# Two groups of a layer accumulated into one second product, GpSimd's work of a layer's first group in another order, a third softmax buffer, and copies of weights and values on ScalarE

## The chip, the cores and the metric

The kernel runs on one core of a Trainium2 chip. The time is device microseconds (us) of one execution, and the median of three runs is what is compared. TensorE (PE) multiplies matrices, VectorE (DVE), ScalarE (ACT) and GpSimd (POOL) work elementwise, SyncE (SP) issues all DMAs here. Each engine works through its own instructions in the written order and waits on semaphores for what others have to finish.

## What is computed

```python
def _attn_ref(q, k, v):                      # 4 x 8 heads, 576 positions, head size 64
    window = 128
    scores = 1.0 / np.sqrt(D) * np.matmul(q, k.transpose(0, 1, 3, 2))
    ...
    mask = (rel >= 0) & (rel < window)
    scores = np.where(mask, scores + bias[None], -1000000000.0)
    scores = scores - np.max(scores, axis=-1, keepdims=True)
    attn = np.exp(scores)
    attn = attn / (np.sum(attn, axis=-1, keepdims=True) + 1e-09)
    return np.matmul(attn, v)

def _moe_ref(x, w_gate, w_val, w_out):       # 2304 tokens, 512 -> 1536 -> 512
    gate = 1.0 / (1.0 + np.exp(-(x @ w_gate)))
    val = x @ w_val
    return gate * val @ w_out

def _moe2_ref(x, w1, w2, w3, w_out):         # 512 -> 1024 -> 1024 -> 512
    a = x @ w1
    b = x @ w2
    h = a * b @ w3
    return h @ w_out
```

The output is `_moe2_ref(_moe_ref(attention))`, in float32. Below, the two feed-forward parts are called layer 1 and layer 2.

## The kernel before

Every float32 operand is split into a high part (`..._hi`, the value cast to the type that PE multiplies quickly, made on ACT) and a low part (`..._lo`, value minus high part, made on DVE or POOL), and a product is three matmuls: high by high, low by high, high by low (`product`, L573).

**Head, 0 to about 134 us.** Attention for the first third of the tokens, 28 steps in `SLOTS` = 36 slots. A step n goes `scores` (PE), `score` (DVE: bias, mask and maximum, from PSUM into `soft[n % 2]`, `negmax`), `exponentials` (ACT), `reciprocals` (DVE), `normalise` (POOL, on `soft`), `turn` (PE: transposes), `turned_hi`/`turned_lo` (ACT, DVE), `pv` (PE: times the values), `out_copy` (ACT). The same slots multiply w3 by layer 2's w_out once (64 `fold`s of three matmuls, L634) so that layer 2 needs one product less; w3 comes in 16 halves, each cast to `w3_hi` on DVE (L1099), its low part from DVE (L1103) or POOL (L1325) in turn. `values_hi` (L981, L983) is on DVE too. The last eight folds follow the slots.

**Body.** Three passes of 768 tokens (two halves of 384), in each six groups of layer 1 (group = 256 hidden columns) and four of layer 2, 30 groups in all. A group has sections: `gate` and `val` (its two first products) and, one group late, `proj`, the second product. The last group of a layer has two `proj` sections, one for the group before and one for itself. `SECTIONS` lists them, 30 to a pass, and every engine runs through that list with its own order of jobs inside a section. One attention step of the next third is placed in each section of the first two passes: `scores(n)` at the section's start, `turn` and `pv` of the step before inside it.

- A first product is a Strassen-like scheme: 2 by 2 blocks with seven multiplications P1, P5, P6, P2, P7, P3, P4, in that order, each of six 128x384 matmuls (`multiply`, L656). It needs sums of weight blocks (`weight_sums`, L1269 to L1277, POOL), their high parts (`weights_hi`, L810 and L812, ACT) and their low parts (`plain_lo`, L1283, and `sums_lo`, L1290, POOL) in two buffers: 0 for gate, 1 for val. It also needs seven sums of input blocks with high and low parts (`xs_hi`, `xs_lo`), made once per layer and pass, when the layer before is finished (`x_sum`, `x_hi`, `x_lo`; `WHOLE` says how many second-product tiles each waits for).
- The result blocks C11, C22, C12, C21 are gated and multiplied on DVE and ACT, and split into `h_hi`, `h_lo` (`h_split` counts the finished blocks of a group; C21 is the last).
- `project(g, k)` (L691) makes one of eight output tiles of group g: six matmuls into one of two PSUM banks. `add_up(g, k)` (L1072; a copy, L1070, in a layer's first group) adds it to `xf` in SBUF. Tile t starts when `acc_done` says that tile t-2 was taken out. `O_TILES` orders the tiles (c: half of the tokens, o: block of output columns).
- Low parts of attention's next inputs, `k_lo`, `q_lo` (L1208, L1215) and `v_lo` (L1226), are in POOL's `splits`, one section ahead of their use for k and q. `out_lo` (L1296, POOL) is the low part of w_out for the group.

At a pass's end SP stores `xf` (L501) and then issues the loads of the next groups.

Of the kernel before, what the change touches and what calls it, by code (L numbers as in the profile page):

```python
# [79 lines left out]
FOLDS_IN = [[k for k in range(NFOLD - IB) if fold_slot(k) == s] for s in range(SLOTS)]  # L80
W3_LOAD_SLOT = {1 + 2 * h: h for h in range(2, HALVES)}
# [33 lines left out]

SECTIONS = []
for g_ in range(NG):
    SECTIONS += [(g_, "gate", g_), (g_, "val", g_)]
    if not first_of(g_):
        SECTIONS.append((g_, "proj", g_ - 1))  # L120
    if last_of(g_):
        SECTIONS.append((g_, "proj", g_))
PASS_SECTIONS = len(SECTIONS) // NPASS

# [94 lines left out]
def build(nc, qT, kT, v, bias8, ident, w3t, wo2, w_gate, w_val, w_out, w1, w2, outT):  # L219
    scratch = nc.dram_tensor("w3_times_wout", (IB, P, DM), F32, kind="Internal").ap()  # L220
    ctx = ExitStack()
    with ctx:
# [23 lines left out]
        xt = [sb(ctx, f"xt{k}", [P, 2 * TH], F32) for k in range(3)]  # L246
# [13 lines left out]
        soft = [sb(ctx, f"soft{b}", [P, 2 * KW], F32) for b in range(2)]  # L260
# [8 lines left out]
        with ExitStack() as one:  # L269
# [7 lines left out]
            w3_raw = sb(one, "w3_raw", [P, IB * P], F32)  # L277
# [16 lines left out]
        w3_in = [sem("w3_in0"), sem("w3_in1")]  # L294
# [4 lines left out]
        v_hi_head, v_hi_done, v_split = sem("v_hi_head"), sem("v_hi_done"), sem("v_split")  # L299
# [100 lines left out]
        def acc_cols(g, c, o):  # L400

            start = o * 2 * TP + g // GP % 2 * TP + c * TH
            return slice(start, start + TH)


        O_TILES = [(0, 0), (0, 1), (1, 0), (1, 1), (1, 2), (1, 3), (0, 2), (0, 3)]

        WHOLE = {P1: 2, P5: 4, P6: 6, P7: 6, P3: 6, P2: 8, P4: 8}

        def wait_x(eng, inst, j):  # L410

            if inst % 2:
                eng.wait_ge(acc_done, 8 * (first_group(inst) - 1) + WHOLE[j])
# [11 lines left out]
        def _(sp):  # L425
            def load_w3(hf):
                if hf >= 2:
                    w3_half_split(sp, hf - 1)
                sp.dma_start(w3_raw[:, w3_cols(hf)], w3t[hf // 2, :, w3_cols(hf)]).then_inc(w3_in[hf % 2], 16)
# [983 lines left out]
```

## Time and profile before

| | us |
|---|---|
| median of 3 runs (1017.22, 1018.2, 1023.16) | 1018.2 |
| the profiled execution's own time | 1019.72 |
| its span, first to last instruction | 1017.9 |
| PE busy | 919.8 (90%) |
| PE weight loads busy | 855.0 (84%) |
| POOL busy | 737.3 (72%) |
| DVE busy | 602.1 (59%) |
| ACT busy | 549.9 (54%) |
| mean granted clock of PE | 0.971 |

PE has 98.1 us of idle time in the span. Views of the trace used here: the list of waits (who sat idle, until which instruction of which engine ended, in total, how often, the longest), the groups of instructions, the instructions of one line, the order of time, and busy times by stretch. In the order of time a row's last bracket is the engine's idle time ahead of it and what ended it. The granted clock is a share of full speed (2.4 GHz); 0.5 is 1.2 GHz.

### The profile page before, as it was taken

To read this page: it belongs to the slowest core of one execution; us is meant where nothing else is said; L and a number is where in the kernel's file an instruction comes from. 1 tells how busy PE (TensorE), PEld (TensorE's weight loads), DVE (VectorE), ACT (ScalarE), POOL (GpSimd) and SP (SyncE) were. 2 spreads that over 40 slices of the span, in tenths; PEclk is the share of its full clock that TensorE was granted. 3 is DMA by queue.
4 is the path that set the end of the run, shared out by engine and by line. 5 is a ranking of instruction groups with operands and counts; after the bars stand their busy time and mean duration, and the time that the engine had idled before them with its cause. 6 is when DMAs were issued, how large, how long until landed. Compare 5 with 4: busy or idle time off the path is not lost.

```text
span 1017.9 us, 16149 instructions
## 1 busy us (share of the span) xinstructions
PE 919.8 (90%) x5352; PEld 855.0 (84%) x5352; DVE 602.1 (59%) x1364; ACT 549.9 (54%) x1259; POOL 737.3 (72%) x626
## 2 busy tenths in 40 slices
PE   3899798999996999978999997799987999987998
PEld 2676587999995899878998996799977999977998
DVE  4657564566666555644665657465574555684555
ACT  4657576666674654446665774565534344334330
POOL 3657998877866986678778775877856877749750
PEclk9999998999998999989999999999998999998999
DMA  6334222323121311042221221122104211112101
GB/s 204 120 104 153 74 96 81 99 89 99 49 82 37 101 62 57 24 148 80 94 83 60 68 76 49 63 92 74 48 10 156 83 63 63 62 42 83 63 21 63
DMA packets 46050, 80.81 MB, mean 79 GB/s; under 512 B 4112, under 2 KB 27280, under 8 KB 45968
## 3 DMA queue, kind: packets, MB, share of 16 engines
q1 hardware_dynamic: 45968, 79.77, 23.4%
q8 instruction: 44, 0.72, 0.3%
q14 instruction: 38, 0.31, 0.1%
HBM read 72.94 MB, written 6.82 MB: 78 GB/s over the span
## 4 chain that ended last, share of the span: by engine, by line
PE 71%; POOL 13%; DVE 7%; issue 4%; DMA 2%; ACT 1%; SPq 1%; DVEq 0%; POOLq 0%; ACTq 0%
PE quad_ps L576 13%; PE quad_ps L578 12%; PE quad_ps L577 12%; PE o_ps L576 8%; PE o_ps L578 7%; PE o_ps L577 7%; POOL wq_lo L1290 2%; PE attn_ps L599 2%; PE attn_ps L576 2%; PE attn_ps L614 2%; POOL xs_lo L1254 2%; DMA wo_lo_raw<-w_out 2%; POOL wq_lo L1283 1%; POOL soft L1239 1%; DVE xf L1072 1%
## 5 line engine op out<-in xcount | busy, mean ns | idle before, releaser
L576 PE MATMUL quad_ps<-xs_hi,wq_hi 128*128 128x384 f32 x840 | 296.8, 353 | 36.4 <-POOL wq_lo L1290 17.8
L578 PE MATMUL quad_ps<-xs_hi,wq_lo 128*128 128x384 f32 x840 | 287.7, 342 | 0.0
L577 PE MATMUL quad_ps<-xs_lo,wq_hi 128*128 128x384 f32 x840 | 287.2, 342 | 0.0
L576 PEld LDWEIGHTS quad_ps<-xs_hi,wq_hi 128*128 128x128 f32 x840 | 163.0, 194 | 44.3 <-POOL wq_lo L1290 19.8
L576 PE MATMUL o_ps<-h_hi,wo_hi 128*128 128x384 f32 x480 | 167.0, 348 | 10.5 <-DVE xf L1072 10.0
L577 PEld LDWEIGHTS quad_ps<-xs_lo,wq_hi 128*128 128x128 f32 x840 | 163.1, 194 | 0.0
L578 PEld LDWEIGHTS quad_ps<-xs_hi,wq_lo 128*128 128x128 f32 x840 | 162.1, 193 | 0.0
L578 PE MATMUL o_ps<-h_hi,wo_lo 128*128 128x384 f32 x480 | 161.5, 337 | 0.0
L577 PE MATMUL o_ps<-h_lo,wo_hi 128*128 128x384 f32 x480 | 161.3, 336 | 0.0
L1021 DVE TENSOR_TENSOR u<-quad_ps,s 128x384 f32<-128x384 f32 x60 | 33.5, 558 | 196.6 <-PE quad_ps L578 195.2
L1290 POOL TENSOR_TENSOR wq_lo<-wsum,wq_hi 128x1024 fp32r<-128x1024 f32 x60 | 143.5, 2392 | 7.7
L1239 POOL TENSOR_TENSOR soft<-soft,recip 128x512 f32<-128x512 f32 (+2 forms) x80 | 73.4, 918 | 96.0 <-DVE recip L965 95.8
L1072 DVE TENSOR_TENSOR xf<-o_ps,xf 128x384 f32<-128x384 f32 x192 | 105.5, 554 | 58.1 <-PE o_ps L578 56.7
L1283 POOL TENSOR_TENSOR wq_lo<-raw_q,wq_hi 128x768 fp32r<-128x768 f32 x60 | 110.6, 1843 | 36.4 <-ACT wq_hi L810 36.4
L576 PEld LDWEIGHTS o_ps<-h_hi,wo_hi 128*128 128x128 f32 x480 | 90.0, 188 | 21.9 <-issue 19.3
L771 ACT ACTIVATE soft<-soft,negmax 128x256 f32<-128x256 f32 (+2 forms) x160 | 75.0, 470 | 52.3 <-DVE negmax L954 52.2
L843 ACT CAST h_hi<-quad_ps 128x384 fp32r<-128x384 f32 x120 | 57.3, 478 | 83.2 <-DVE quad_ps L1055 82.6
L577 PEld LDWEIGHTS o_ps<-h_lo,wo_hi 128*128 128x128 f32 x480 | 90.2, 188 | 0.0
L578 PEld LDWEIGHTS o_ps<-h_hi,wo_lo 128*128 128x128 f32 x480 | 90.1, 188 | 0.0
L824 ACT COPY s<-quad_ps 128x384 f32<-128x384 f32 x60 | 28.8, 481 | 112.2 <-PE quad_ps L578 112.1
L1296 POOL TENSOR_TENSOR wo_lo<-wo_lo_raw,wo_hi 128x1024 fp32r<-128x1024 f32 x30 | 71.8, 2394 | 19.6 <-ACT wo_hi L818 19.6
L837 ACT ACTIVATE sig<-quad_ps 128x384 f32<-128x384 f32 x120 | 58.1, 491 | 39.3 <-DVE quad_ps L1044 14.9
(91 smaller groups left out, 1807.4 us busy)
## 6 DMA issues: line engine op xcount, KB each, us to landing
raw_q<-w SPq DMA_DIRECT2D x24, 512.0 KB, 3.5
raw_q<-w_gate SPq DMA_DIRECT2D x18, 512.0 KB, 3.5
raw_q<-w_val SPq DMA_DIRECT2D x18, 512.0 KB, 4.5
wo_lo_raw<-w_out SPq DMA_DIRECT2D x18, 512.0 KB, 3.5
wo_lo_raw<-w_times_wout SPq DMA_DIRECT2D x12, 512.0 KB, 3.7
w_raw<-w3t SPq DMA_DIRECT2D x16, 256.0 KB, 2.7
q_lo_raw<-qT SPq DMA_DIRECT2D x16, 192.0 KB, 3.8
bias<-bias SPq DMA_DIRECT2D x12, 256.0 KB, 4.5
```

Of the source, the lines that this page charges most:

```text
L576: pe.matmul(out, lh, rh, start=start, stop=False, skip_group_check=onto)
L577: pe.matmul(out, lh, rl, start=False, stop=False, skip_group_check=onto)
L578: return pe.matmul(out, ll, rh, start=False, stop=stop, skip_group_check=onto)
L771: op = nc.scalar.activation(cols, cols, ACT.Exp, scale=-1.0, bias=negmax[0:rows, 2 * buf + h:2 * buf + h + 1], accum_out=rowsum[0:rows, 2 ...
L837: nc.scalar.activation(sig[:, piece(blk)], quad[BANK_OUT[blk]][:, 0:TH], func).then_inc(gated, 1)
L843: nc.scalar.copy(h_hi[g % 2][:, piece(blk)], quad[BANK_OUT[blk]][:, 0:TH]).then_inc(h_hi_done, 1)
L1021: nc.vector.tensor_tensor(out=u2[:, :], in0=quad[1][:, 0:TH], in1=s1[:, :], op=ALU.add).then_inc(u2_done, 1)
L1072: op = nc.vector.tensor_tensor(out=xf[:, cols], in0=ps_o[t % 2][:, 0:TH], in1=xf[:, cols], op=ALU.add)
L1239: nc.gpsimd.tensor_tensor(out=cols, in0=cols, in1=recip[0:rows, 2 * buf:2 * buf + 2].unsqueeze(2).to_broadcast([rows, 2, keys.stop - keys. ...
L1283: nc.gpsimd.tensor_tensor(out=wq_lo[m][:, 0:PLAIN], in0=raw_q[m][:, GW:GW + PLAIN], in1=wq_hi[m][:, 0:PLAIN], op=ALU.subtract).then_inc(wq ...
L1290: nc.gpsimd.tensor_tensor(out=wq_lo[m][:, PLAIN:7 * GW], in0=wsum[m][:, :], in1=wq_hi[m][:, PLAIN:7 * GW], op=ALU.subtract).then_inc(wq_sp ...
L1296: nc.gpsimd.tensor_tensor(out=wo_lo[g % 2][:, :], in0=wo_raw[g % 2][:, :], in1=wo_hi[g % 2][:, :], op=ALU.subtract).then_inc(wo_split, 1)
```

## The change

1. **Second products of a layer's last two groups together.** The two last `proj` sections become `pair0` and `pair1`. `pair0` makes tiles 0 to 3 for both groups, `pair1` tiles 4 to 7, each tile summed over both groups in PSUM and added to `xf` once. `O_TILES` begins with the second token half (c = 1), whose tiles need all blocks up to C21. DVE's and POOL's jobs in these sections are reordered, and so is the order of ACT's `x_hi` there.
2. **POOL's order in the `val` section of a layer's first group**: `plain_lo(g+1, 0)` and `sums_lo(g+1, 0)` stand first, then `normalise`, `weight_sums(g+1, 1)`, the splits, `out_lo(g)` and `plain_lo(g+1, 1)`.
3. **Third `soft` buffer**: `score(n)` waits for `turn(n-3)` and `exponentials(n-2)`, where it waited for `turn(n-2)`.
4. **Head**: `w3_hi` and `values_hi` are made on ACT; `w3_raw` has three half buffers and its loads stand a slot or so earlier (SP issues one more, `load_w3(2)`, in its opening list); folds 56 to 61 are in the last slots and two folds follow them, where eight did. The buffers share memory with `xt1` and `xt2`, so DVE and POOL wait for the last w3 split before `x_sum(0, ...)`.

```diff
-FOLDS_IN = [[k for k in range(NFOLD - IB) if fold_slot(k) == s] for s in range(SLOTS)]
-W3_LOAD_SLOT = {1 + 2 * h: h for h in range(2, HALVES)}
+FOLDS_IN = [[k for k in range(NFOLD) if fold_slot(k) == s] for s in range(SLOTS + 1)]
+W3_LOAD_SLOT = {2 * h - 1: h for h in range(3, HALVES)}
...
+def tiles_to(g):
+
+    return 8 * (project_of(g) + 1) if g >= 0 else 0
...
-        O_TILES = [(0, 0), (0, 1), (1, 0), (1, 1), (1, 2), (1, 3), (0, 2), (0, 3)]
-
-        WHOLE = {P1: 2, P5: 4, P6: 6, P7: 6, P3: 6, P2: 8, P4: 8}
+        O_TILES = [(1, 0), (1, 1), (0, 0), (0, 1), (1, 2), (1, 3), (0, 2), (0, 3)]
+
+        WHOLE = {P1: 4, P5: 4, P6: 6, P7: 6, P3: 6, P2: 8, P4: 8}
...
+            def project(e, k, g):
+
+                start, stop = g == PROJECTS[e][0], g == PROJECTS[e][-1]
+                c, o = O_TILES[k]
+                t, hb = 8 * e + k, g % 2
...
                 pe.wait_ge(h_split, 4 * g + 1 + max(HALF_OF[0][c], HALF_OF[1][c]))
-                wait(pe, acc_done, t - 1)
+                if start:
+                    wait(pe, acc_done, t - 1)
...
+                        lo = 4 * (kind == "pair1")
+                        parts = [(lo + k, of) for k, of in ((0, g - 1), (1, g - 1), (0, g), (1, g),
+                                                            (2, g - 1), (3, g - 1), (2, g), (3, g))]
...
+                if s in W3_HI_SLOT:
+                    hf = W3_HI_SLOT[s]
+                    act.wait_ge(w3_in[hf % 3], 16 * (hf // 3 + 1))
+                    wait(act, fold_half, hf - 1)
+                    nc.scalar.copy(w3_hi[:, w3_cols(hf)], w3_raw[hf % 3][:, :]).then_inc(w3_hi_done, 1)
+                for j in range(HEAD_JOBS):
+                    if s == FIRST[j] + 6:
+                        values_hi(j)
...
-                        for j in (P6, P7, P2, P3, P4):
+                        for j in (P6, P3, P7, P2, P4):
                             x_hi(inst, j)
...
                 dve.wait_ge(qk_done, n + 1)
-                wait(dve, turned, n - 1)
+                wait(dve, turned, n - 2)
+                wait(dve, exp_done, n - 1)
...
+                elif kind == "val" and first_of(g):
+                    plain_lo(g + 1, 0)
+                    sums_lo(g + 1, 0)
+                    if n is not None:
+                        normalise(n)
+                    weight_sums(g + 1, 1)
+                    splits(sec)
+                    out_lo(g)
+                    plain_lo(g + 1, 1)
```

GpSimd, in the `val` section of the first group and the `gate` section after it (group 0; groups 6 and 16 have the same rows with other sizes). `wq_lo0` is for the next gate section, `wq_lo1` for the next val section, `k_lo1`, `q_lo1` for the scores at the start of that val section. Before:

```order
L1226 TENSOR_TENSOR v_lo0<-v_lo0_raw,v_hi0 128x512 [waits v_hi_done]
L1296 TENSOR_TENSOR wo_lo0<-wo_lo0_raw,wo_hi0 128x1024 [waits wo_hi_done]
L1269 TENSOR_TENSOR wsum1<-raw_q1 128x256 [waits wq_split1,rawq_in1]
L1271 TENSOR_TENSOR wsum1<-raw_q1 128x256
L1274 TENSOR_TENSOR wsum1<-wsum1,raw_q1 128x256 [waits wsum_done1]
L1277 TENSOR_TENSOR wsum1<-raw_q1,wsum1 128x256 [waits wsum_done1]
L1239 TENSOR_TENSOR soft1<-soft1,recip 128x512 [waits recip_done]
L1283 TENSOR_TENSOR wq_lo0<-raw_q0,wq_hi0 128x768 [waits wq_hi_done0]
L1290 TENSOR_TENSOR wq_lo0<-wsum0,wq_hi0 128x1024 [waits wq_plain0,wq_hi_done0]
L1283 TENSOR_TENSOR wq_lo1<-raw_q1,wq_hi1 128x768 [waits wq_hi_done1]
L1290 TENSOR_TENSOR wq_lo1<-wsum1,wq_hi1 128x1024 [waits wq_plain1,wq_hi_done1]
L1269 TENSOR_TENSOR wsum0<-raw_q0 128x256 [waits wq_split0,rawq_in0]
```

Now:

```order
L1251 TENSOR_TENSOR v_lo0<-v_lo0_raw,v_hi0 128x512 [waits v_hi_done]
L1308 TENSOR_TENSOR wq_lo0<-raw_q0,wq_hi0 128x768 [waits wq_hi_done0]
L1315 TENSOR_TENSOR wq_lo0<-wsum0,wq_hi0 128x1024 [waits wq_plain0,wq_hi_done0]
L1264 TENSOR_TENSOR soft2<-soft2,recip 128x512 [waits recip_done]
L1294 TENSOR_TENSOR wsum1<-raw_q1 128x256 [waits wq_split1,rawq_in1]
L1296 TENSOR_TENSOR wsum1<-raw_q1 128x256
L1299 TENSOR_TENSOR wsum1<-wsum1,raw_q1 128x256 [waits wsum_done1]
L1302 TENSOR_TENSOR wsum1<-raw_q1,wsum1 128x256 [waits wsum_done1]
L1321 TENSOR_TENSOR wo_lo0<-wo_lo0_raw,wo_hi0 128x1024 [waits wo_hi_done]
L1308 TENSOR_TENSOR wq_lo1<-raw_q1,wq_hi1 128x768 [waits wq_hi_done1]
L1315 TENSOR_TENSOR wq_lo1<-wsum1,wq_hi1 128x1024 [waits wq_plain1,wq_hi_done1]
L1294 TENSOR_TENSOR wsum0<-raw_q0 128x256 [waits wq_split0,rawq_in0]
```

The low parts for the next gate section moved from the seventh and eighth place of this stretch to the first two behind `v_lo0`, ahead of w_out's (`wo_lo0`) and of the sums `wsum1`. What follows row `wsum0`, up to `q_lo1`, stands as it did.

VectorE, at the section in which the last group of layer 1 (group 5) is multiplied by w_out for the first time. `quad_ps3` is block C21, `h_lo1` the low parts of this group. Before:

```order
L1072 TENSOR_TENSOR xf<-o_ps0,xf 128x384 [waits o_done]
L1055 TENSOR_TENSOR quad_ps3<-quad_ps3,sig 128x384 [waits gated,c21_done]
L1072 TENSOR_TENSOR xf<-o_ps1,xf 128x384 [waits o_done]
L1060 TENSOR_TENSOR h_lo1<-quad_ps1,h_hi1 128x384 [waits h_hi_done]
L1072 TENSOR_TENSOR xf<-o_ps0,xf 128x384 [waits o_done]
L1060 TENSOR_TENSOR h_lo1<-quad_ps3,h_hi1 128x384 [waits h_hi_done]
L972 TENSOR_TENSOR pt_lo0<-attn_ps0,pt_hi0 128x256 [waits pt_hi_done]
L965 RECIPROCAL recip<-rowsum2 128x2 [waits norm_done,sum_done]
L1072 TENSOR_TENSOR xf<-o_ps1,xf 128x384 [waits o_done]
L1072 TENSOR_TENSOR xf<-o_ps0,xf 128x384 [waits o_done]
L1072 TENSOR_TENSOR xf<-o_ps1,xf 128x384 [waits o_done]
```

Now:

```order
L1087 TENSOR_TENSOR h_lo1<-quad_ps1,h_hi1 128x384 [waits h_hi_done]
L992 ISA soft2,negmax<-attn_ps0,bias0 128x256 [waits exp_done,turned,qk_done]
L992 ISA negmax 128x1
L992 ISA soft2,negmax<-attn_ps1,bias0 128x256
L992 ISA negmax 128x1
L1082 TENSOR_TENSOR quad_ps3<-quad_ps3,sig 128x384 [waits gated,c21_done]
L1087 TENSOR_TENSOR h_lo1<-quad_ps3,h_hi1 128x384 [waits h_hi_done]
L1010 TENSOR_TENSOR pt_lo0<-attn_ps0,pt_hi0 128x256 [waits pt_hi_done]
L1003 RECIPROCAL recip<-rowsum2 128x2 [waits norm_done,sum_done]
L1098 TENSOR_TENSOR xf<-o_ps0,xf 128x384 [waits o_done]
L1098 TENSOR_TENSOR xf<-o_ps1,xf 128x384 [waits o_done]
L1098 TENSOR_TENSOR xf<-o_ps0,xf 128x384 [waits o_done]
L1098 TENSOR_TENSOR xf<-o_ps1,xf 128x384 [waits o_done]
```

The low part of C12 moved ahead of the score and that of C21 ahead of all additions, and the section has four additions instead of eight.

VectorE, in the section that closes layer 1 (`xt0`, `xt1` are input sums of the next layer, `xs_lo` their low parts). Before:

```order
L1072 TENSOR_TENSOR xf<-o_ps0,xf 128x384 [waits o_done]
L1072 TENSOR_TENSOR xf<-o_ps1,xf 128x384 [waits o_done]
L1072 TENSOR_TENSOR xf<-o_ps0,xf 128x384 [waits o_done]
L972 TENSOR_TENSOR pt_lo0<-attn_ps0,pt_hi0 128x512 [waits pt_hi_done]
L965 RECIPROCAL recip<-rowsum2 128x2 [waits norm_done,sum_done]
L1072 TENSOR_TENSOR xf<-o_ps1,xf 128x384 [waits o_done]
L1007 TENSOR_TENSOR xt0<-xf 128x768 [waits xs_split6,acc_done]
L1072 TENSOR_TENSOR xf<-o_ps0,xf 128x384 [waits o_done]
L1072 TENSOR_TENSOR xf<-o_ps1,xf 128x384 [waits o_done]
L1007 TENSOR_TENSOR xt1<-xf,xt0 128x768 [waits t_done6,t_done1,xs_split2,acc_done]
L1013 TENSOR_TENSOR xs_lo<-xt0,xs_hi 128x768 [waits xs_hi_done1]
L1072 TENSOR_TENSOR xf<-o_ps0,xf 128x384 [waits o_done]
```

Now:

```order
L1034 TENSOR_TENSOR xt0<-xf 128x768 [waits xs_split6,acc_done]
L1010 TENSOR_TENSOR pt_lo0<-attn_ps0,pt_hi0 128x512 [waits pt_hi_done]
L1003 RECIPROCAL recip<-rowsum2 128x2 [waits norm_done,sum_done]
L1040 TENSOR_TENSOR xs_lo<-xt0,xs_hi 128x768 [waits xs_hi_done1]
L1098 TENSOR_TENSOR xf<-o_ps0,xf 128x384 [waits o_done]
L1098 TENSOR_TENSOR xf<-o_ps1,xf 128x384 [waits o_done]
L1034 TENSOR_TENSOR xt1<-xf,xt0 128x768 [waits t_done6,t_done1,xs_split2,acc_done]
L1098 TENSOR_TENSOR xf<-o_ps0,xf 128x384 [waits o_done]
L1040 TENSOR_TENSOR xs_lo<-xt1,xs_hi 128x768 [waits xs_hi_done2]
L1098 TENSOR_TENSOR xf<-o_ps1,xf 128x384 [waits o_done]
```

One input sum and its low part, which waits for ACT's high part (`xs_hi_done`), moved ahead of the first addition of the section.

## Rows read from the trace of the kernel before

**Rows 1.** Waits of PE, whole span: total us, times, longest.

```profile
PE quad_ps L576 <- POOL wq_lo L1290: 17.8, 5, 4.6
PE attn_ps L614 <- DVE negmax L954: 12.7, 2, 7.0
PE quad_ps L576 <- ACT sig L837: 10.6, 3, 5.2
```

**Rows 2.** POOL in order of time, the first layer change, groups 6 and 7.

```profile
337.53 2.40 POOL L1296 TENSOR_TENSOR wo_lo<-wo_lo_raw,wo_hi 128x1024 fp32r<-128x1024 f32 x1
...
343.79 1.83 POOL L1283 TENSOR_TENSOR wq_lo<-raw_q,wq_hi 128x768 fp32r<-128x768 f32 x1
345.76 2.37 POOL L1290 TENSOR_TENSOR wq_lo<-wsum,wq_hi 128x1024 fp32r<-128x1024 f32 x1
...
357.40 1.02 POOL L1215 TENSOR_TENSOR q_lo<-q_lo_raw,q_hi 128x384 fp32r<-128x384 f32 x1
```

**Rows 3.** ACT's line L810 there: two casts, ns, first and last start in us.

```profile
L810 ACT CAST wq_hi<-raw_q x2: 834/834/835, 340.0 to 345.8; 128x768 fp32r<-128x768 f32 x2
```

**Rows 4.** PE in order of time at the same layer change.

```profile
348.18 0.69 PE L576 MATMUL quad_ps<-xs_hi,wq_hi 128*128 128x384 f32 x1 [2.41 <-POOL wq_lo L1290]
348.67 0.52 PE L577 MATMUL quad_ps<-xs_lo,wq_hi 128*128 128x384 f32 x1
348.99 0.52 PE L578 MATMUL quad_ps<-xs_hi,wq_lo 128*128 128x384 f32 x1
...
353.34 0.33 PE L576 MATMUL quad_ps<-xs_hi,wq_hi 128*128 128x384 f32 x1
353.52 0.33 PE L577 MATMUL quad_ps<-xs_lo,wq_hi 128*128 128x384 f32 x1
...
358.52 0.33 PE L599 MATMUL attn_ps<-k_hi,q_hi 64*128 64x128 f32 x2
```

**Rows 5.** Stretch of 10 us: PE busy, granted clock, DMA share, GB/s.

```profile
770.00:780.00 10.00, 6.14 (x24) 0.66 0.16 64
```

**Rows 6.** ACT and POOL in order of time, start of pass 0, group 0.

```profile
147.96 2.42 POOL L1296 TENSOR_TENSOR wo_lo<-wo_lo_raw,wo_hi 128x1024 fp32r<-128x1024 f32 x1
148.64 0.84 ACT L810 CAST wq_hi<-raw_q 128x768 fp32r<-128x768 f32 x1
...
168.68 1.02 POOL L1215 TENSOR_TENSOR q_lo<-q_lo_raw,q_hi 128x384 fp32r<-128x384 f32 x1
```

**Rows 7.** ACT and PE in order of time, start of pass 1, groups 10 and 11.

```profile
450.03 1.04 ACT L818 CAST wo_hi<-wo_lo_raw 128x1024 fp32r<-128x1024 f32 x1 [6.61 <-DMA wo_lo_raw<-w_out]
453.02 0.66 PE L576 MATMUL quad_ps<-xs_hi,wq_hi 128*128 128x384 f32 x1 [4.65 <-ACT sig L837]
459.62 0.83 ACT L810 CAST wq_hi<-raw_q 128x768 fp32r<-128x768 f32 x1
467.77 0.69 PE L576 MATMUL quad_ps<-xs_hi,wq_hi 128*128 128x384 f32 x1 [3.62 <-POOL wq_lo L1290]
```

**Rows 8.** PE in order of time, third layer change, no attention left.

```profile
934.52 0.44 PE L576 MATMUL quad_ps<-xs_hi,wq_hi 128*128 128x384 f32 x1 [3.08 <-POOL wq_lo L1290]
```

**Rows 9.** PE and DVE in order of time: a second product's section from its start.

```profile
418.27 0.34 PE L576 MATMUL o_ps<-h_hi,wo_hi 128*128 128x384 f32 x1
...
422.29 0.55 DVE L1060 TENSOR_TENSOR h_lo<-quad_ps,h_hi 128x384 fp32r<-128x384 f32 x1
```

**Rows 10.** Groups of instructions, 0 to 134 us: busy, mean ns, idle before.

```profile
L954 DVE CUSTOM_DVE_ANT_0 soft<-quad_ps,bias 128x256 f32<-128x256 f32 (+2 forms) x56 | 18.2, 361 | 37.3 <-PE quad_ps L614 37.3
L1099 DVE CAST w_hi<-w_raw 128x512 fp32r<-128x512 f32 x16 | 11.3, 709 | 9.1 <-DMA w_raw<-w3t 9.1
L876 ACT CAST wo_hi<-wo_lo_raw 128x512 fp32r<-128x512 f32 x8 | 4.7, 613 | 5.1 <-DMA wo_lo_raw<-wo 5.1
```

**Rows 11.** Busy PE, PEld, DVE, ACT, POOL, granted clock, DMA; the head.

```profile
0.00:134.00 134.00, 103.70 (x600) 78.55 (x600) 80.23 (x240) 82.40 (x270) 89.81 (x102) 0.97 0.39 124
```

**Rows 12.** PE's waits, 20 to 134 us: total, times, longest.

```profile
PE o_ps L576 <- POOL w_lo L1325: 7.3, 6, 2.1
```

More of the change, by code:

```diff
@@ L116, with project_of @@
 SECTIONS = []
+PROJECTS = []
 for g_ in range(NG):
[L118 to L120 removed]
+    SECTIONS += [(g_, "gate"), (g_, "val")]
     if last_of(g_):
[L122 removed]
+        SECTIONS += [(g_, "pair0"), (g_, "pair1")]
+        PROJECTS.append((g_ - 1, g_))
+    elif not first_of(g_):
+        SECTIONS.append((g_, "proj"))
+        PROJECTS.append((g_ - 1,))
 PASS_SECTIONS = len(SECTIONS) // NPASS
+def project_of(g):
+    return [e for e, groups in enumerate(PROJECTS) if g in groups][0]
+def tiles_to(g):
+    return 8 * (project_of(g) + 1) if g >= 0 else 0
 def step_at(sec):
@@ L722, in _ @@
                     scores(n)
-                if kind == "proj":
-                    for k in range(8):
-                        project(of, k)
-                        if k == 1 and m is not None:
-                            turn(m)
-                        if k == 5 and m is not None:
-                            pv(m)
-                else:
+                if kind in ("gate", "val"):
                     for j in range(7):
@@ L735, in _ @@
                         if j == P7 and m is not None:
+                            pv(m)
+                else:
+                    e = project_of(g - 1)
+                    if kind == "proj":
+                        parts = [(k, g - 1) for k in range(8)]
+                    else:
+                        lo = 4 * (kind == "pair1")
+                        parts = [(lo + k, of) for k, of in ((0, g - 1), (1, g - 1), (0, g), (1, g),
+                                                            (2, g - 1), (3, g - 1), (2, g), (3, g))]
+                    for i, (k, of) in enumerate(parts):
+                        project(e, k, of)
+                        if i == 1 and m is not None:
+                            turn(m)
+                        if i == 5 and m is not None:
                             pv(m)
@@ L1136, in _ @@
                     result_21(2 * g)
+                    if more and g % GP == GP - 1:
+                        x_sum(inst, P5)
                 elif kind == "val":
@@ L1162, in _ @@
                     for k in range(3, 8):
-                        add_up(of, k)
-                    if more and g % GP == GP - 1:
-                        x_sum(inst, P5)
-                        x_lo(inst, P5)
-                elif g % GP == G1 - 1:
-                    for k in range(3):
-                        add_up(of, k)
+                        add_up(e, k)
+                elif kind == "pair0":
+                    hidden(g, C21)
+                    hidden_lo(g, C21)
                     if m is not None:
```

218 lines of the change are left out of this document (109 added, 109 removed).

## The prediction

> **What bounds the kernel now.** The page comes first: PE is busy for 90% of the span and idle for 98.1 us, so the time can only change by what happens to these gaps, since the change keeps PE's matmuls as they are (96 for the last two groups of a layer before and after, the same 64 folds). The list of PE's waits then says who ends the gaps [rows 1]. The largest term is POOL's `wq_lo` at L1290, 17.8 us in five waits (4.61 at the start of pass 0, 2.41, 4.12 and 3.08 at the three changes from layer 1 to layer 2, 3.62 at the start of pass 1); `negmax`, 12.7 in two, and `sig`, 10.6 in three, are the input chains of a layer change and of a pass start. Last the order of time around one of the five [rows 2 to 4]: POOL, not PE, is full there. From 337.53 to the end of `q_lo` at 358.42 it has no idle time, and PE's next scores start at 358.52, 0.10 us behind that end. So the wait of 2.41 us is not the only thing that POOL holds up: PE comes to the next waiting place exactly when POOL has finished its whole list.
>
> **The cost of a stop.** Behind a gap the matmuls come every 0.32 us, against 0.18 us once the clock is back [rows 4]; a stretch with such a gap has a granted clock of 0.66 [rows 5], a mix of the two levels 1.2 and 2.4 GHz. Twelve matmuls at 0.32 instead of 0.18 cost 1.7 us. A stop is therefore its length plus about 1.7 us, where it is over some 2.4 us long and no cover follows.
>
> **Part 2, POOL's order.** At the first layer change, now, `plain_lo(g+1, 0)` waits for ACT's cast, which starts at 339.98 (shown as 340.0) and takes 0.83 [rows 3], and that cast stands behind PE's and ACT's work, which doesn't move. Before, `out_lo` and the weight sums filled POOL's time until then. Now POOL is idle from 337.58 to 340.87, 3.3 us, and then does the same instructions, 358.42 - 337.53 = 20.9 us of them, to 361.8. The `wq_lo` wait goes (ready at 340.87 + 4.3 = 345.2; 4.3 is from 343.79 to the end of the row at 345.76 [rows 2]; PE comes at 348.18 - 2.41 = 345.8), but the next scores wait for `q_lo` until 361.8 instead of 358.5: -3.3. PE comes there with the stop of about 6 us in front and a cold clock behind: -1.7. Together **-5.0**. The second layer change (group 16) has the same pattern, PE's wait being 4.12 there; I take the same **-5.0**.
>
> Start of pass 0 [rows 6]: POOL would be free at 147.96, the cast ends at 149.48, idle 1.5. Some of it may be given back before `q_lo` ends at 169.70, since that is 21.7 us for the work that took 20.9 at the layer change: 0.8 to 0.9 us of it looks like slack, so -0.6, between 0 and -1.5, and -1.7 for the clock. Start of pass 1 [rows 7]: there the cast is late for another reason, below. Third layer change [rows 8]: no attention is left, so no `q_lo` to wait for. The 3.08 us at 934.52 go, and PE's next stop, for the val weights, is worked out from POOL's list: the low parts for gate ended at about 934.5; with sums and `out_lo` (2.9 + 2.4) behind them they would end at 929.2, a little later if the cast is late, and I take 930.7. Then sums, `out_lo` and the next low parts, 2.9 + 2.4 + 4.3 = 9.6, to 940.3. PE comes at 931.4 + 7.3 (42 matmuls) = 938.7 and stops for 1.6; before, it started that section at 934.5 + 7.3 + 1.7 = 943.5: **+3.2**.
>
> **Part 1, pairs.** The section starts with tiles that need C21. Of group g-1 these are there; 12 matmuls later (2.08 us) it is group g's turn. In a section without attention steps C21's low part was the third thing of DVE, 422.29 + 0.55 = 422.8, 4.6 us after the section's start at 418.27 [rows 9]; without the two additions ahead of it (0.93) and with ACT's high part before it, I take 3.7. PE stops for 3.7 - 2.08 = 1.6 us. That is so at the six layer ends: at four of them the time is given back, because PE waited for the input chain or the loads behind anyway (7.03 us at the first change [rows 1], 4.65 at a pass start [rows 7]); at the last it is lost, **-1.65**. Half the additions fall away there: 8 for each of six ends, all beside PE's matmuls. At the two layer changes with attention I let the chain of the next inputs come out the same, with one stop more ahead of it inside the 7.03 us (section 2's first addition now stands behind `x_lo`, which waits for ACT): **0**, between -2 and +2 each, bounded by the 1.9 us of an `x_lo` more or less.
>
> At a pass end the shared tiles are complete about 3.5 us earlier, because the last section's additions don't wait behind input sums any more; so the store, the loads behind it, ACT's `wo_hi` at 450.03 and PE's 453.02 [rows 7] come 3.5 us earlier. But in pass 1 POOL's new order then lies ahead of `q_lo`: cast at 459.62 - 3.6, ready 456.85; low parts 4.3, `normalise` and sums 3.9 (from 337.53 + 2.35 to 343.79 [rows 2]), `k_lo` and `q_lo` 2.0: 466.9, then 0.5 for the scores, against 467.77 before: **+0.35**. In pass 2 (a gap of 5.2 us by the list [rows 1]) 3.4 come, and 1.5 are given back to the low parts of val: **+1.9**.
>
> **Parts 3 and 4, head.** PE is busy 103.7 of 134 us, ACT 82.4, POOL 89.8 [rows 11]. DVE's score waits for PE's transposes 37.3 us in 24 places, 1.55 each [rows 10]; a third buffer takes that wait away, so that exponentials, `normalise` and everything behind them on POOL come up to 1.55 us earlier in a slot. The waits for `w_lo` (7.3 in six [rows 12]) shrink by about 4.7 (each by up to 1.55); of the rest of the head's 134 - 103.7 = 30.3 us without matmuls, most of it loads at the start, I take 3.8 for waits in the slots: 8.5. Against it: ACT gets 16 casts of 0.61 [rows 10] and 12 of values at about as much, 17.7 us, on top of 82.4, which leaves it 34 us of slack over the head but little at its fullest: -1.5. G = **+7** with the startup as it is. The bounds are 0 (ACT eats all) and +11. Six of the last folds now stand ahead of the last `pv`, from which the input sums hang: up to 3.9 us, of which I take 2.0 as seen at the start of pass 0: **-2.0**. A page of the Trainium skill bears on the casts: SBUF — State Buffer, Who interferes with whom, says that a DVE copy or cast in its two-port mode locks out GpSimd for the whole instruction, and ACT locks nobody out. The row for `w_hi` on DVE has a mean of 709 ns where ACT's for the same shape has 613 [rows 10]; that doesn't tell whether a lock is in it. By that rule POOL would gain up to the casts' own 11.3 us more than I count; my sum leaves it out.
>
> **The sum.** 7.0 - 2.0 - 0.6 - 1.7 (head and start) - 5.0 - 5.0 + 0.35 + 1.9 + 3.2 - 1.65 = -3.5, that is 3.5 us slower: 1019.7 + 3.5 = 1023.2 against the profiled execution's own time. The median of the three runs is 1.5 below that execution, so the forecast is **1021.7**.
>
> **Rivals.**
> A. *The waits for `wq_lo` go and nothing takes their place.* 17.8 us, the clock behind four of them, 4 x 1.3 (nine matmuls), and the head's 5, less the end's 1.65: 26 us, 992 to 1000. For it: the list of waits [rows 1]. Against it: POOL has no slack up to `q_lo` [rows 2]. It decides where `q_lo` ends: if POOL finds other work for the 3.3 us. The Trainium skill, Perfetto Trace Analysis, Optimization Strategy, would have one look for the gaps of the most contended engine and make their dependencies start sooner; taken alone it gives this rival. Chance 0.17.
> B. *ACT becomes the head's bound* (the side of slower by over 1%). If the 17.7 us that ACT gets lie on the chain score, exp, `recip`, `normalise` for more than 13 of them, the 7 turn into -6 or worse: 1021.7 + 7 + 0 to 6 = 1029 to 1035. For it: the copies stand in ACT's order between two steps. Against it: ACT has 51.6 us free there. Chance 0.17.
> C. *The gaps move and cost nothing more*, because the clock doesn't fall behind the new stop, or because POOL's idle time is filled: 3 x 1.7 less, 1014 to 1018. Chance 0.22.
> My forecast, 1018 to 1027: 0.44.
>
> **How the numbers follow.** The range that leaves out no more than 2 in 10 takes C, the forecast, the lower half of B and the nearest part of A: 1003 to 1031; the likeliest case's own is 1018 to 1027. One per cent, 10.2 us, is about what a measurement of this kernel can tell from no change. Under 1008: A and a little of C, 0.2. Over 1028.4: B, 0.17. Between: 0.63.
>
> **What would show it.** In PE's waits: `quad_ps <- wq_lo` falls from 17.8 to under 4, and `attn_ps <- q_lo` appears with three or four waits of about 6 us (step of part 2; if it is absent, A). POOL waits for ACT's cast ahead of `plain_lo` 3.3 us at the first layer change. `o_ps <- h_lo` six times 1.6 us in the pair sections (part 1). In the head `o_ps <- w_lo` falls below 3 us and ACT is busy 18 us more; DVE is busy some 47 us less over the span. If the first input sums come later than 130 us, the head's gain is not there (B). The forecast is wrong by most if scores at the layer changes don't wait.

## The result and the profile after

The changed kernel takes 1038.21 us (median of four runs, 1036.08 to 1039.21), the one before 1019.33 (four runs): a ratio of 1.0178, 95% interval 1.0142 to 1.0214. It is 18 to 19 us slower where 3.5 us were forecast, and outside the range of 1003 to 1031.

The page of the changed kernel, first part, and the list of PE's waits over the span (who waited for whom: total us, times, longest). L618 are the scores (L599 before), L595 the first matmul of a product (L576 before):

```profile
PE 932.4 (90%) x5352; PEld 867.3 (84%) x5352; DVE 559.1 (54%) x1280; ACT 562.4 (54%) x1295; POOL 736.5 (71%) x627
```

```profile
PE attn_ps L618 <- issue: 18.2, 7, 7.2
PE quad_ps L595 <- ACT sig L866: 12.1, 3, 5.2
PE attn_ps L633 <- DVE negmax L992: 11.2, 4, 4.0
PE o_ps L595 <- DVE xf L1098: 10.8, 11, 3.5
PE o_ps L595 <- POOL w_lo L1350: 10.0, 5, 3.9
PE quad_ps L595 <- ACT s L853: 9.1, 5, 3.7
...
PE quad_ps L595 <- POOL wq_lo L1315: 0.9, 2, 0.5
```

The 17.8 us of `wq_lo` [rows 1] are 0.9 now, as part 2 meant. In their place stand the scores (18.2 in seven, where they were 1.6 in three; the list says "issue", since what PE waited for, `q_lo`, had ended within the last tenth of a microsecond) and a wait for `s`, the copy of a result block that ACT makes in the middle of a first product: 9.1 in five, where it was 3.5 in one. PE does the same 5352 matmuls in 932.4 us of busy time instead of 919.8: the mean granted clock is 0.957 instead of 0.971. So three quarters of the 16.3 us by which the span grew (1034.2 against 1017.9) are matmuls at the slower clock; PE's idle time grew by only 3.7.

The starts of the first product's sections in the two traces (first matmul of each `gate` and `val`, in the order of time) say where the difference arises. "Later by" is after minus before, and each row's own part is the step from the row above.

| up to | later by | own part | forecast |
|---|---|---|---|
| start of group 0 (head) | -0.3 | -0.3 | -5.0 |
| group 2 (start of pass 0) | 4.4 | +4.7 | +2.3 |
| group 8 (first layer change) | 10.4 | +6.0 | +5.0 |
| val of group 11 (start of pass 1) | 11.7 | +1.3 | -0.35 |
| group 18 (second layer change) | 17.3 | +5.6 | +5.0 |
| group 21 (end of pass 1, start of pass 2) | 22.3 | +5.0 | -1.9 |
| group 28 (third layer change) | 17.1 | -5.2 | -3.2 |
| end of the span | 16.3 | -0.8 | +1.65 |

Two rows carry most of the error: the head, 4.7 us, and the end of pass 1, 6.9 us. The forecast's -5.0 in the head row is a gain of 7.0 less a loss of 2.0 for the folds, and that loss was expected at the start of pass 0. A loss of that size does arise there, in the next row: the first gate section takes 11.5 us instead of 8.8 (11.8 in e9, which has the early folds and no cast on ScalarE). With the 2.0 moved to that row, the head misses by 6.7 and the start of pass 0 by 0.4.

Each step comes from one trace of each kernel. Sections without a wait repeat within 0.05 us; the head, with the same instructions, differs by 2.4 us between the trace of the kernel before and that of e1. In medians the miss is 16.5 us (1038.2 against 1021.7) where the table has 12.8: the profiled execution of the changed kernel, 1036.1, was its fastest, and the forecast had been set 1.5 below the profiled one of the kernel before.

**The first layer change, after.** POOL in the order of time (start, duration, line, what; the last bracket is its idle time ahead and who ended it), and PE's two stops there:

```profile
341.35 1.29 POOL L1251 TENSOR_TENSOR v_lo<-v_lo_raw,v_hi 128x512 fp32r<-128x512 f32 x1
346.18 1.85 POOL L1308 TENSOR_TENSOR wq_lo<-raw_q,wq_hi 128x768 fp32r<-128x768 f32 x1 [3.54 <-ACT wq_hi L839]
...
365.92 0.99 POOL L1243 TENSOR_TENSOR q_lo<-q_lo_raw,q_hi 128x384 fp32r<-128x384 f32 x1
```

```profile
356.37 0.45 PE L595 MATMUL quad_ps<-xs_hi,wq_hi 128*128 128x384 f32 x1 [1.48 <-ACT s L853]
...
367.01 0.47 PE L618 MATMUL attn_ps<-k_hi,q_hi 64*128 64x128 f32 x2 [5.06 <-issue]
...
368.33 0.52 PE L596 MATMUL quad_ps<-xs_lo,wq_hi 128*128 128x384 f32 x1
368.65 0.52 PE L597 MATMUL quad_ps<-xs_hi,wq_lo 128*128 128x384 f32 x1
```

POOL stands idle for 3.54 us where it did `out_lo` and sums before [rows 2], and then needs 20.7 us without a pause (20.9 before) from 346.18 to the end of `q_lo` at 366.9; the scores start at 367.01. Behind that stop matmuls come every 0.32 us again.

**The wait for `s`.** ACT in the order of time, same place:

```profile
351.10 0.84 ACT L839 CAST wq_hi<-raw_q 128x768 fp32r<-128x768 f32 x1
354.51 1.05 ACT L841 CAST wq_hi<-wsum 128x1024 fp32r<-128x1024 f32 x1 [2.58 <-POOL wsum L1302]
355.46 0.47 ACT L872 CAST h_hi<-quad_ps 128x384 fp32r<-128x384 f32 x1
355.84 0.48 ACT L853 COPY s<-quad_ps 128x384 f32<-128x384 f32 x1
```

In the new order the weight sums for val come on POOL behind the low parts for gate. ACT's cast of these sums (`weights_hi(g+1, 1)`) waits for them, and `keep`, which makes `s`, is queued behind it on ACT. PE waits for `s` in the middle of the gate section. The forecast had not followed the moved weight sums to that cast.

**The end of pass 1.** DVE, PE and POOL in the order of time:

```profile
745.36 5.04 DVE L1034 TENSOR_TENSOR xt<-xf 128x768 f32<-128x768 f32 x1
750.33 0.34 DVE L992 CUSTOM_DVE_ANT_0 soft<-attn_ps,bias 64x192 f32<-64x192 f32 x1
```

```profile
751.10 1.09 PE L633 MATMUL attn_ps<-eye,soft 128*128 128x128 f32 x4 [3.45 <-DVE negmax L992]
```

```profile
745.15 2.39 POOL L1321 TENSOR_TENSOR wo_lo<-wo_lo_raw,wo_hi 128x1024 fp32r<-128x1024 f32 x1
747.51 0.72 POOL L1294 TENSOR_TENSOR wsum<-raw_q 128x256 f32<-128x256 f32 x1
748.19 0.72 POOL L1296 TENSOR_TENSOR wsum<-raw_q 128x256 f32<-128x256 f32 x1
748.87 0.72 POOL L1299 TENSOR_TENSOR wsum<-wsum,raw_q 128x256 f32<-128x256 f32 x1
749.66 1.32 POOL L1302 TENSOR_TENSOR wsum<-raw_q,wsum 128x256 f32<-128x256 f32 x1
```

The change had also moved an input sum of the next pass (`x_sum(inst, P5)`; the five others of its kind take 0.95 to 1.14 us) into the last gate section of a pass. Here it took 5.04 us (5.01 in e3's trace, which has it at the same place), and the score of the next step, which PE's transposes wait for, stood behind it.

**The head.** POOL's waits from 20 to 134 us:

```profile
POOL soft L1264 <- DVE recip L1003: 15.0, 8, 4.0
POOL v_lo L1251 <- ACT v_hi L791: 12.4, 7, 2.5
POOL v_lo L1251 <- ACT v_hi L789: 6.3, 4, 2.1
```

and POOL in the order of time at one of PE's stops (2.66 us, ended at 61.55 by `w_lo`, L1350):

```profile
58.16 0.73 POOL L1251 TENSOR_TENSOR v_lo<-v_lo_raw,v_hi 128x256 fp32r<-128x256 f32 x1 [2.33 <-ACT v_hi L791]
58.85 0.46 POOL L1254 TENSOR_TENSOR v_lo<-v_lo_raw,v_hi 64x128 fp32r<-64x128 f32 x1
59.27 1.00 POOL L1243 TENSOR_TENSOR q_lo<-q_lo_raw,q_hi 128x384 fp32r<-128x384 f32 x1
60.22 1.27 POOL L1350 TENSOR_TENSOR w_lo<-w_raw,w_hi 128x512 fp32r<-128x512 f32 x1
```

POOL waits 18.7 us for the values' high parts (3.4 before), which ACT makes at the end of a slot, behind exponentials and `turned_hi`. `w_lo`, which PE's folds wait for, is queued behind. PE's waits for `w_lo` from 20 to 134 us are 6.1 us in all; they were 7.3 [rows 12], and less than 3 were forecast.

### The profile page after: what moved, and what is told of

Read it like the earlier page. It is cut to its first block and busy times, and to the rows that moved or that the text cites. A ratio compares the mean times of both kernels' runs of the same rounds, so it can differ in the third digit from the quotient of the medians.

```text
span 1034.2 us, 16072 instructions
## 1 busy us (share of the span) xinstructions
PE 932.4 (90%) x5352; PEld 867.3 (84%) x5352; DVE 559.1 (54%) x1280; ACT 562.4 (54%) x1295; POOL 736.5 (71%) x627
## 5 line engine op out<-in xcount | busy, mean ns | idle before, releaser
L595 PE MATMUL quad_ps<-xs_hi,wq_hi 128*128 128x384 f32 x840 | 299.3, 356 | 23.7 <-ACT sig L866 12.1
L595 PEld LDWEIGHTS quad_ps<-xs_hi,wq_hi 128*128 128x128 f32 x840 | 164.4, 196 | 33.1 <-issue 17.0
L595 PE MATMUL o_ps<-h_hi,wo_hi 128*128 128x384 f32 x480 | 168.1, 350 | 11.3 <-DVE xf L1098 10.8
L1264 POOL TENSOR_TENSOR soft<-soft,recip 128x512 f32<-128x512 f32 (+2 forms) x80 | 75.6, 946 | 80.0 <-DVE recip L1003 79.8
L1098 DVE TENSOR_TENSOR xf<-o_ps,xf 128x384 f32<-128x384 f32 x144 | 79.1, 554 | 69.7 <-PE o_ps L597 68.9
L595 PEld LDWEIGHTS o_ps<-h_hi,wo_hi 128*128 128x128 f32 x480 | 91.4, 190 | 21.1 <-issue 18.7
```

What stands on the lines that cost most here:

```text
L595: pe.matmul(out, lh, rh, start=start, stop=False, skip_group_check=onto)
L1098: op = nc.vector.tensor_tensor(out=xf[:, cols], in0=ps_o[t % 2][:, 0:TH], in1=xf[:, cols], op=ALU.add)
L1264: nc.gpsimd.tensor_tensor(out=cols, in0=cols, in1=recip[0:rows, 2 * buf:2 * buf + 2].unsqueeze(2).to_broadcast([rows, 2, keys.stop - keys. ...
```

## The experiments

The three suspects (GpSimd's order, the values' casts on ScalarE, the input sum) were undone one at a time, then together; each was also approached from another side. Times are medians; each ratio is against the kernel before on the same chip.

**Part 2 alone (e1).** On the kernel before, only GpSimd's section changed:

```diff
+                elif kind == "val" and first_of(g):
+                    plain_lo(g + 1, 0)
+                    sums_lo(g + 1, 0)
                 elif kind == "val":
...
                     normalise(n)
+                if kind == "val" and first_of(g):
+                    weight_sums(g + 1, 1)
                 splits(sec)
                 if kind == "val" and first_of(g):
-                    plain_lo(g + 1, 0)
-                    sums_lo(g + 1, 0)
+                    out_lo(g)
                     plain_lo(g + 1, 1)
```

> The kernel before with part 2 alone (GpSimd's order in the val section of a layer's first group). My theory from the two traces: the wait for wq_lo at L1290 falls from 17.8 us to about 1, the scores behind it wait for q_lo instead (about 4, 5 and 5 us at the start of pass 0 and at two layer changes, 7 at the start of pass 1), and the clock falls behind each stop; the third layer change gains about 5. In sum 8 to 10 us slower than before, about 1028. Rival, that the order is harmless and the loss of 19 us lies in the pair sections and the head: within 3 us of before.

Measured: 1037.3 us, ratio 1.0181 (1.0143 to 1.0220). The rival is out: the order alone costs as much as the whole change, so the rest of the change gains in some places what it loses in others. The size was more than the 8 to 10 expected; its profiled execution has a span of 1031.1, 13.2 longer, and the runs spread from 1033 to 1041. By the section starts, the order alone costs 2.2 us at the start of pass 0, 5.4 at the first layer change, 5.8 at the start of pass 1 and 4.2 at the second layer change, and gives 1.1 at the third. Its list of PE's waits has the scores in first place:

```profile
PE attn_ps L599 <- issue: 17.2, 6, 6.6
...
PE quad_ps L576 <- ACT s L824: 7.8, 5, 2.5
PE attn_ps L599 <- POOL k_lo L1208: 7.2, 2, 5.5
```

**Part 2 undone (e2).** The changed kernel with the old order in that branch:

```diff
                 elif kind == "val" and first_of(g):
+                    out_lo(g)
+                    weight_sums(g + 1, 1)
+                    if n is not None:
+                        normalise(n)
+                    splits(sec)
                     plain_lo(g + 1, 0)
                     sums_lo(g + 1, 0)
-                    if n is not None:
-                        normalise(n)
-                    weight_sums(g + 1, 1)
-                    splits(sec)
-                    out_lo(g)
                     plain_lo(g + 1, 1)
```

> The changed kernel with GpSimd's old order in that section, everything else as changed. My theory: 8 to 10 us faster than the changed kernel, 1028 to 1030, with the wq_lo waits back and no score waiting for q_lo at the layer changes. Rival: the order was harmless, 1036 to 1039.

Measured: 1023.08 us, 1.0048 (1.0031 to 1.0065). So 1.0178 falls by 1.3 points, 13 us, more than the 8 to 10 expected. The scores' "issue" waits are 1.6 us in three again, and the `wq_lo` waits are back:

```profile
PE quad_ps L595 <- POOL wq_lo L1315: 18.0, 5, 4.6
```

**Why the order costs: `q_lo` earlier (e5).** The changed kernel with its new order, and in the section after it:

```diff
+                if kind == "gate" and g and first_of(g - 1):
+                    sums_lo(g, 1)
+                    splits(sec)
+                    if n is not None:
+                        normalise(n)
+                    weight_sums(g + 1, 0)
```

where weight sums and `normalise` stood ahead of `splits` (the low parts of keys and queries).

> The changed kernel with one more move on GpSimd: in the gate section of a layer's second group, the low parts of the next keys and queries go ahead of normalise and of the weight sums (about 3 to 4 us of work) that stood before them. It tests why the new order of part 2 costs 15 us. My theory: it costs because GpSimd is the bound up to q_lo and the new order gives it idle time ahead of ScalarE's cast; then q_lo is ready 3 to 4 us earlier at four places, the stops there shrink from 4 to 7 us to 0 to 3 and most of the cold clock goes: 1024 to 1029. Rival: the stops come from something else behind q_lo, such as the keys' and queries' high parts or their loads, and stay: 1036 to 1039.

Measured: 1019.95 us, 1.0007 (0.9993 to 1.0020). One move, of two instructions of 1 us each (`normalise` also comes ahead of the weight sums), takes back 17 of the 18 us; theory and direction hold, and the gain is above the range that I gave (1024 to 1029). At the first layer change the stop is 1.25 us and the clock stays up:

```profile
356.66 1.00 POOL L1243 TENSOR_TENSOR q_lo<-q_lo_raw,q_hi 128x384 fp32r<-128x384 f32 x1
```

```profile
357.75 0.33 PE L618 MATMUL attn_ps<-k_hi,q_hi 64*128 64x128 f32 x2 [1.25 <-issue]
```

The first score takes 0.33 us here, and 0.47 behind the stop of 5.06 us. The theory named four places. By the section starts the gain is 5.8, 5.7 and 5.0 us at the start of pass 0 and at the first two layer changes, but only 0.6 at the start of pass 1: there the scores still stop for 6.2 us, because the `q_lo` that they wait for is made in the val section, which this edit doesn't touch. The wait for `s` is unchanged in this run (9.1 us in five), so it is not what made the 18 us; what it costs by itself was not tried.

**The values' casts back on VectorE (e3).** In the head `values_hi(j)` goes from ScalarE's slots to VectorE's, as before the change; the casts of w3 stay on ScalarE.

```diff
-                act.wait_ge(v_in[st], 16 * value_loads_to(j))
...
-                op = nc.scalar.copy(v_hi[st][:, 0:full], v_raw[st][:, 0:full])
+                dve.wait_ge(v_in[st], 16 * value_loads_to(j))
...
+                op = nc.vector.tensor_copy(v_hi[st][:, 0:full], v_raw[st][:, 0:full])
```

> The changed kernel with the head's casts of values (12 full ones and 8 short ones) back on VectorE; the casts of w3 stay on ScalarE. In the changed kernel GpSimd waits 18.8 us in the head for these casts on ScalarE (3.4 us before for the ones on VectorE), and the lead of 2.9 us that the third buffer gives by step 8 is gone by step 21. My theory: GpSimd's wait falls under 5 us, the lead stays, and the body starts 3 to 6 us earlier: 1032 to 1035. Rival, that PE itself is the bound of the head from 65 us on, so that no lead can be kept: 1037 to 1039, same start of the body within 1 us.

Measured: 1026.56 us, 1.0075 (1.0046 to 1.0103), 11 us less than the changed kernel, beyond the 3 to 6 expected. The body starts at 123.9 instead of 134.5. PE was not the bound of the head. POOL's waits, 20 to 134 us:

```profile
POOL soft L1278 <- DVE recip L1000: 18.5, 12, 2.7
POOL wq_lo L1322 <- ACT wq_hi L839: 2.4, 1, 2.4
POOL v_lo L1265 <- DVE v_hi L1018: 2.4, 6, 0.9
...
POOL v_lo L1265 <- DVE v_hi L1016: 0.9, 3, 0.3
```

18.7 us of waits for values are 3.3, as they were before the change.

**The third buffer alone (e8).** The kernel before with part 3:

```diff
-                wait(dve, turned, n - 1)
+                wait(dve, turned, n - 2)
+                wait(dve, exp_done, n - 1)
```

> The kernel before with the third softmax buffer alone. In the changed kernel with the values' casts on VectorE the body starts at 123.9 us against 134.8 before; the question is how much of that is the buffer. My theory: the buffer gives most of it, 6 to 9 us, since VectorE's score waited 37.3 us for transposes: 1010 to 1013. Rival: the w3 casts on ScalarE and the early folds give it, the buffer alone 0 to 3.

Measured: 1010.86 us, 0.9917 (0.9896 to 0.9938): 8.5 us, within the forecast of the experiment. PE's waits from 20 to 134 us: those for `w_lo`, 7.3 before [rows 12], are

```profile
PE o_ps L576 <- POOL w_lo L1326: 1.8, 3, 0.8
```

The body starts at 125.7 in it and at 123.9 in e3, so all that the w3 casts on ScalarE and the early folds can add to the start is 2 us. The first gate section is longer with them (9.2 us against 7.5, up to the scores behind it), and at its end the two stand within 0.1 us: nothing of it is left.

**The input sum behind the gate section (e4), and one job earlier (e10).** The changed kernel with `x_sum(inst, P5)` taken from the end of the last gate section; in e4 it goes into `pair0`, in e10 it moves up by one job:

```diff
+                    if more and g % GP == GP - 1:
+                        x_sum(inst, P5)
                     result_21(2 * g)
-                    if more and g % GP == GP - 1:
-                        x_sum(inst, P5)
```

> The changed kernel with one VectorE job moved: the first input sum of the next pass (L1034, 128x768, both inputs in SBUF), which the change had moved into the gate section of a pass's last group, goes to the section behind it (pair0, after the reciprocals). In the changed kernel that sum took 5.04 us at 745.36 beside GpSimd's work, and the scores of the last step waited behind it (PE idle 3.45 us, then a cold clock). My theory: this stop goes and the kernel is 4 to 5 us faster, 1033 to 1034, all of it in the last gate and val sections of pass 1. Rival: the stop only moves into the pair section, 1037 to 1039.

> The changed kernel with the first input sum of the next pass moved by one VectorE job only, ahead of the last result block of the gate section, where GpSimd is idle or at its casts. It tells the place from the competition with GpSimd: in the changed kernel the sum took 5.04 us beside w_out's low part and the weight sums. Theory, it took so long because GpSimd's instructions kept it from its second reading: at the earlier place, where GpSimd waits for ScalarE, it takes 1 to 2 us, and the kernel gains 3 to 5 us, 1033 to 1035. Rival, the sum is long wherever it stands in this section: 1037 to 1039.

Measured: e4 1032.78 us, 1.0139 (1.0118 to 1.0159); e10 1030.87 us, 1.0109 (1.0090 to 1.0129). Both take the stop away: e4 gains 5.4 us (4 to 5 expected), e10 7.3 (3 to 5 expected), and their intervals overlap. In e4 the end of pass 1 makes -1.4 us against the kernel before, where the table has +5.0 and the forecast had -1.9. In e10 the sum is in the same section and right next to its old place, and takes a quarter of the time; it begins 1.5 us before `out_lo` does:

```profile
744.30 1.25 DVE L1034 TENSOR_TENSOR xt<-xf 128x768 f32<-128x768 f32 x1
```

So the sum is not long wherever it stands in this section; what differs at the two places is what POOL does beside it.

**All three undone (e6).** 

> The changed kernel with the three suspects undone together: GpSimd's old order in the val section of a layer's first group, the values' casts of the head on VectorE, the first input sum behind the gate section. Alone they gave 15.1, 11.7 and 5.4 us against the changed kernel. My theory, they lie at different places (starts of layers and pass 0; the head; the last gate section of pass 1) and add up: 1038.2 - 32.2 = 1006. Rival, they share a bound: 1012 to 1018.

Measured: 1008.60 us, 0.9886 (0.9852 to 0.9921). The sum of the single effects, 1006, holds within the interval (about 1004 to 1011); the three lie at different places.

**What is left without the buffer (e9).** e6, with `soft` back to two buffers and the w3 casts on VectorE; left are the pair sections and the early loads and folds.

> The variant with the three suspects undone, and without the third softmax buffer and with the w3 casts back on VectorE too; what is left of the change is the pair sections and the early loads and folds of the head. Theory: the buffer gave 8.5 us alone, so this is about 1017, that is the pairs give 0 to 3 us against before. Rival, that the pairs cost (their stops at tiles that need C21 and the addition behind an input sum): 1020 to 1024.

Measured: 1017.28 us, 0.9973 (0.9956 to 0.9991). The pair sections, with the early loads and folds, bring about 3 us (the interval says 1 to 4.5). By the section starts they cost 0.3 us at the first layer change and 3.1 at the second, and give 1.9 and 2.1 around the two pass changes and 3.9 at the third layer change. That is one trace, of this kernel's fastest run; but e2, the changed kernel with the old order, has 3.8 at the second layer change too.

**Better orders (e7, e11) and the same without pairs (e12).** e7 is e6 with `out_lo`, `plain_lo`, `sums_lo`, `normalise`, `weight_sums`, `splits`, `plain_lo` in the val section, so that POOL has work until the cast, and e5's gate section. e11 is e7 with `splits` in second place. e12 has both sections of e7 and the third buffer on the kernel before, nothing else.

> The same with another order on GpSimd: in the val section of a layer's first group w_out's low part fills the time until ScalarE's cast, then the low parts for the next gate section, then normalise and the weight sums; and in the gate section after it keys and queries stand ahead of normalise and weight sums. Theory: neither a wait for wq_lo nor one for q_lo is left at the layer changes; that is up to 17 us less than the variant with the old order: 990 to 1000. Rival: the work that was put back (normalise, weight sums) becomes the next wait: 1003 to 1008.

> The best variant so far (1001.6) with the keys' and queries' low parts ahead of the gate's low parts in the val section of a layer's first group too. At the start of pass 1 the scores of group 11 still wait 7.1 us there. Theory: the stop shrinks to under 4 us, 5 us with the clock, 996 to 998. Rival: it becomes a wait for wq_lo of the same length, 1000 to 1003.

> The kernel before, with only the third softmax buffer and GpSimd's orders of the variant that took 1001.6 us: no pair sections, no casts moved to ScalarE, folds as before. Theory: the pairs and the w3 casts are worth 0 to 4 us, so 1001 to 1006. Rival, the pairs cost more than they bring: 995 to 1000.

Measured: e7 1001.59 us, 0.9826 (0.9804 to 0.9847); e11 999.29 us, 0.9805 (0.9779 to 0.9831); e12 1003.54 us, 0.9839 (0.9819 to 0.9860). e7 is faster than e6 by 7 us, where the theory wanted up to 17; it lies between the two expectations, nearer the rival: at the start of pass 1 a stop of 7.1 us is left and the wait for `s` came along. e11, too, lies between its two expectations (996 to 998, and 1000 to 1003), and e12 within its theory (1001 to 1006). Between e7, e11 and e12 the intervals overlap. In the section starts e11 gains 6.3 us on e7 between the start of group 10 and the val section of group 11, and gives 3.8 back by group 17, where it waits 4.1 us for `wq_lo` again. The best of these is about 20 us faster than the kernel before, and 16 of them are there without the pairs and without any cast moved to ScalarE.

## The prediction, point by point

- **What bounds, and part 2: right in the mechanism and in the places, too small in sum.** The `wq_lo` waits go, POOL idles ahead of ScalarE's cast (3.3 us forecast, 3.54 seen), `q_lo` becomes the end that PE waits for, the clock falls behind. PE stops at the scores four times, for 3.9, 5.1, 7.2 and 5.4 us (three or four of about 6 forecast), so rival A is out, and e5 shows that an earlier `q_lo` takes the cost away at three of the four. The sizes agree partly by luck. The start of pass 0, put at 2.3, is 4.7, of which 2.6 are the first gate section, that is part 4; the order alone makes 2.2 (e1). The second layer change, put at 5.0, is 5.6, but the order alone makes 4.2 there (e1) and the pairs 3.1 (e9), where the forecast had 0 for them. The first, put at 5.0, is 6.0 (order alone 5.4). At the start of pass 1 the order alone costs 5.8 (e1); the forecast had about 3 for it, its +0.35 being that and the 3.5 of the earlier loads. What the moved weight sums add, through ScalarE's cast and `s`, was not separated.
- **Parts 3 and 4, head: the first step that failed.** "ACT gets 16 casts ... and 12 of values ..., 17.7 us ... -1.5." I summed ScalarE's busy time and asked for room. The casts of w3 did fit. But the values' casts have someone who waits for them, POOL's `v_lo`, and in POOL's queue `w_lo` stands behind. The term for the buffer, 8.5, was right (e8: 8.5); with the values on VectorE it is all there (e3: the body starts 10.6 us earlier than in the changed kernel). So the term of -1.5 for the casts measures about -10.5, in time of the kernel too (1.0178 to 1.0075). ScalarE is busy 11 us more in the head, not 18. The 2.0 for the folds came as the longer first gate section. It is rival B's place, with another mechanism: ACT was never full (93.4 of 134 us busy), it was late. Whether the same casts earlier in ScalarE's slots would have been in time was not tried. That POOL gains up to 11.3 us when the w3 casts leave VectorE doesn't show: e8, with them there, and e3, without, are level at the end of the first gate section.
- **Part 1, the move that I left out: the second step that failed.** `x_sum(inst, P5)` into the last gate section appears in the diff and in no sentence of the forecast. It made +5.0 of what was to be -1.9 at the pass change; without it the step is -1.4 (e4), so the term itself was about right. The -3.6 us at the other pass change came: group 10 starts 4.0 us earlier relative to group 9.
- **The stops in the pair sections, 1.6 us each: wrong.** PE's waits for `h_lo` are 0.4 us in all; C21's low part was in time. At the end of the span, where -1.65 was put, nothing is lost: the table's -0.8 is in e1 as well, which has no pairs. What PE did wait for in the pair sections is the addition behind the input's low part, 3.48 and 2.36 us at the layer changes with attention, where the forecast let the input chain come out the same. At the first the wait of 7.03 us behind it shrinks to 4.03 and one of 1.86 ahead goes, so that it cost next to nothing (0.3 in e9); at the second 5.65 shrinks only to 3.38, and it cost 3.1 (e9), outside the bounds of 2.
- **Third layer change**: -3.2 forecast, -5.2 seen, and the cause is half missed. The forecast gave all of it to the order; the order alone brings 1.1 (e1) and the pairs 3.9 (e9), for which nothing was put here. The stop of 1.6 us for the val weights is 0.4.
- **The clock, 1.7 us per stop**: about right for each (a val section of 8.8 us takes 10.3 behind a stop), but there are more stops, 12.6 us of busy time in all.
- **Slips in the sum**: 4.3 + 3.9 + 2.0 from 456.85 is 467.05, not 466.9, so the term of +0.35 should have been +0.2; 28 casts of 0.61 are 17.1 us, not 17.7; and of the six layer ends the text accounts for five. None of them matters beside the misses above.

## What to carry to other kernels

Before moving work on an engine that has no slack, go to the next place where another engine waits for the end of its list, and not only to the wait that the move is aimed at. Work that fills the time until a late input arrives costs nothing; here the order of first use threw that away. A cast moved to an engine with room in its busy share can still be late: look at what stands ahead of it in that queue, who waits for it, and what is queued behind the one that waits. And every line of a diff that changes a place gets its price, also those that look like bookkeeping.

## What the runs showed of the hardware

A VectorE addition of 128x768 with both inputs in SBUF, 0.95 us with GpSimd idle beside it (at 312.01), took 5.04 us while GpSimd ran five instructions back to back from 745.15 to 750.98, and 1.25 us when it began ahead of them (e10). The last of the five, L1302, took 1.32 us, and 0.73 at the first layer change. That is what one would see if the addition was held off until about 749.4 and then held off GpSimd in turn. The Trainium skill, SBUF — State Buffer, Who interferes with whom, states that a DVE instruction with two SBUF inputs contends with a GpSimd instruction that reads SBUF, and that the port pair which they share is an exclusive lock. The runs agree in kind; in length the wait here went over several GpSimd instructions in a row, not one. That it was this port is argued from the durations; the experiments show only that the same sum in the same section takes 1.25 us with other work of GpSimd beside it.
